# Gate and value projections: two 64-row matmuls on the two row halves of TensorE in place of two 128-row matmuls

## The chip, the cores and the metric

The kernel runs on one core of one Trainium2 chip. The metric is the device time of one execution in microseconds. Three runs of the kernel before took 503.9, 504.02 and 505.62 us; their median is 504.02 us.

## The reference, cut to what matters

```python
x  = attention(q, k, v, i_gate, f_gate, o_gate)   # 1536 tokens x 320, a gated linear attention, chunk by chunk
xn = x / rms(x) * rms_g
g  = xn @ w_gate                                  # 320 x 1536
val = xn @ w_val                                  # 320 x 1536
x  = (g * sigmoid(g) * val) @ w_out               # 1536 x 320
h  = x @ w_in                                     # 320 x 2048
y  = (max(h, 0) + alpha * min(h, 0)) @ w_out2     # 2048 x 320
```

The contraction of the projections is 320 long: two blocks of 128 rows and a remainder of 64 rows. The kernel keeps float32 precision with operands rounded to fp32r: each operand is split into a rounded ("high") part and what is left ("low"), and high x high, high x low and low x high are summed in PSUM. Low x low may be left out.

## The kernel before, in words

The 1536 tokens are worked in four tiles of 384 (`TW`). A tile has an attention part (`ATT`: three groups of 128 tokens, each with the items qT, kT, D0, D1, S, state, inter, intra, norm, scale, xT) and a feed-forward part (`MLP`). `merged()` lays the feed-forward items of tile t and the attention items of tile t+1 into one list; all five engines walk the same list, so the order on TensorE is written out by hand. The first attention tile runs alone (the opening), then three merged tiles, then the last feed-forward part alone.

The feed-forward part of a tile runs over the 12 blocks of 128 hidden columns as gate j, val j, out1 j-1, and then over 16 blocks as in j, out2 j-2. There are thus 4 x 12 = 48 pairs of a gate and its val.

`project` (L964 to 977) makes one such block: eight matmuls of 128 rows x 128 columns against 384 columns of tokens, summed in one PSUM bank (`GV[0]` for gate, `GV[1]` for val). The weights' tile has five blocks. Blocks 0 and 1 are the high parts of the two full 128-row blocks, 2 and 3 their low parts, and block 4 holds the 64-row remainder twice: high part in rows 0 to 63, low part in rows 64 to 127. The tokens' tile `xT[:, part, block, :]` has part 0 high and part 1 low, and its block 2 holds the remainder in both row halves. One pass of block 4 against the high tokens gives high x high and low x high at once. One pass of block 4 against the low tokens gives high x low, which is wanted, and low x low, which is not needed: half of that pass does nothing of use. It is the last of the eight.

After gate j, ScalarE takes the tanh (L532) and VectorE makes `u` (L727); after val j, VectorE makes `hid` (L733), ScalarE rounds it (L510) and GpSimd makes its low part (L845), and `accumulate` (L984, L987) multiplies it by the output weights, nine matmuls of 320 columns. TensorE waits for `s_u` ahead of gate j and for `s_hid` ahead of val j (which frees `GV[1]`).

Between a gate and its val there can be an attention item. In each of the three merged tiles the list puts `gates` behind gate 5 (L891: 8-row matmuls, L894: 40-row transposes), and S behind gate 7 and gate 11 (L928). Item S multiplies `kT` and `qT` for two heads that lie in the two row halves (rows 0 to 39 and rows 64 to 103, the variable `r`), taking turns, eight plain float32 matmuls in all, each of which shows in the trace as two:

```python
for c in range(PAIRS):
    for half in range(2):
        r = HP * half
        last = te.matmul(A[1 - half][:, c * CH:(c + 1) * CH], kT[r:r + D, c, :], qT[r:r + D, c, :], ...)
```

The qT and kT items (L904) are float32 transposes on all 128 rows, 128 columns each.

Of the kernel before, what the change touches and what calls it, by code (L numbers as in the profile page):

```python
# [21 lines left out]
F32 = mybir.dt.float32  # L22
F32R = mybir.dt.float32r
ALU = mybir.AluOpType
# [5 lines left out]
P = 128  # L30
CH = 128
G = 3
TW = G * CH
# [11 lines left out]
NB = DM // P  # L45
REM = DM - NB * P
# [80 lines left out]
def program(nc, q, k, v, i_gate, f_gate, o_gate, w_gate, w_val, w_out, rms_g, w_in, w_out2, alpha, out):  # L127
    ctx = ExitStack()
    with ctx:
        def sb(name, shape, dt=F32):  # L130
            return ctx.enter_context(nc.sbuf_tensor(name, shape, dt))

        def sem(name):
            return ctx.enter_context(nc.semaphore(name))


        wg = sb("wg", [P, 5, FF1], F32R)
        wv = sb("wv", [P, 5, FF1], F32R)
# [13 lines left out]
        xT = sb("xT", [P, 2, XB, TW], F32R)  # L152
# [54 lines left out]
        GV = bank[3:5]  # L207
# [4 lines left out]
        def opening(t):  # L212

            return isinstance(t, int) and t == 0
# [28 lines left out]
        s_wgv_lo = sem("s_wgv_lo")  # L243
# [42 lines left out]
        s_gate_mm = sem("s_gate_mm")  # L286
        s_th1 = sem("s_th1")
        s_u = sem("s_u")
        s_val_mm = sem("s_val_mm")
# [298 lines left out]
        def _(dve):  # L588
            vec = nc.vector
# [176 lines left out]
            def weights(n):  # L766

                if n == EARLY - 1:
                    dve.wait_ge(s_alpha_mm, 1)
                    vec.tensor_copy(alpha_sb[:, :], GV[0][:, 0:J2]).then_inc(s_alpha, 1)  # L770
                if n == 0:
                    return
                n -= 1
                what, c = PIECES[n]
                if what == "o":
                    return
                dve.wait_ge(s_w_hi, n + 1)
                w = wg if what == "g" else wv
                cols = slice(c * SW, (c + 1) * SW)
                src = stage[:, n % NS, :].rearrange("p (a n) -> p a n", a=XB)  # L780
                if what == "g":
                    vec.tensor_tensor(wg[:, NB:2 * NB, cols], src[:, 0:NB], wg[:, 0:NB, cols].bitcast(F32), ALU.subtract)
                vec.tensor_tensor(w[REM:P, 2 * NB, cols], src[REM:P, NB], w[REM:P, 2 * NB, cols].bitcast(F32), ALU.subtract).then_inc(s_wgv_lo, 1)

            tiles(dve, mlp, att, weights)


# [79 lines left out]
        def _(pe):  # L867
            te = nc.tensor
# [9 lines left out]
            def keep(count):  # L878

                for _ in range(count):  # L880
                    te.matmul(quad(GV[1]), identR[:, :], mid(maskR[:, :], P, 4, CH), start=True, stop=True)  # L881
# [79 lines left out]
                        last = te.transpose(xbank(g, t)[:, c * CH:(c + 1) * CH], xn[:, g, c * P:(c + 1) * P], ident[:, :])  # L961
                    last.then_inc(s_x_mm, 1)

            def project(dst, w, x, col, lo=NB, first_of=None, t=None):  # L964


                terms = [(a, 0, a) for a in range(NB)] + [(a, 1, a) for a in range(NB)] + [(lo + a, 0, a) for a in range(NB)]
                terms += [(lo + NB, 0, NB), (lo + NB, 1, NB)]
                terms.sort(key=lambda term: term[1])
                for n, (blk, part, xb) in enumerate(terms):  # L970
                    if part and not terms[n - 1][1]:
                        if first_of == "gate":
                            pe.wait_ge(s_x_lo, BACK + G * t + G)
                        elif first_of == "in":
                            pe.wait_ge(s_x2_lo, G * t + G)
                    last = te.matmul(dst, w[:, blk, col:col + P], x[:, part, xb, :], start=(n == 0), stop=(n == len(terms) - 1))  # L976
                return last

            def accumulate(t, i, w_hi, w_lo, first, final):

                pe.wait_ge(s_hid_hi, BACK + JA * t + i + 1)
                for g in range(G):
                    for m, w in enumerate((w_hi, w_lo)):
                        te.matmul(ACC[g][:, 0:DM], hidT[:, i % NH, 0, g * CH:(g + 1) * CH], w, start=(first and m == 0), stop=False)  # L984
                pe.wait_ge(s_hid_lo, BACK + JA * t + i + 1)
                for g in range(G):
                    last = te.matmul(ACC[g][:, 0:DM], hidT[:, i % NH, 1, g * CH:(g + 1) * CH], w_hi, start=False, stop=final)  # L987
                    if final and g < G - 1:
                        last.then_inc(s_acc_mm, 1)
                last.then_inc(s_out_mm, 1)  # L990

            def mlp(what, j, t):
                if what == "gate":
                    if j * P % SW == 0:
                        pe.wait_ge(s_w_hi, AT[("v", j * P // SW)] + 1)
                        pe.wait_ge(s_wgv_lo, 2 * (j * P // SW) + 2)
                        pe.wait_ge(s_wv_lo, j * P // SW + 1)
                    if j == 0:
                        if opening(t):
                            keep(KEEP_GATE)  # L1000
                        pe.wait_ge(s_alpha, 1)
                        pe.wait_ge(s_x_hi, G * t + G)
                        pe.wait_ge(s_hid, BACK + JA * t)
                    else:
                        pe.wait_ge(s_u, BACK + J1 * t + j)
                    project(GV[0][:, 0:TW], wg, xT, j * P, NB, "gate" if j == 0 else None, t).then_inc(s_gate_mm, 1)
                elif what == "val":
                    if j:
                        pe.wait_ge(s_hid, BACK + JA * t + j)
                    project(GV[1][:, 0:TW], wv, xT, j * P).then_inc(s_val_mm, 1)  # L1010
                elif what == "out1":
                    if j % SJ == 0:
                        pe.wait_ge(s_w_hi, AT[("o", j // SJ)] + 1)
                        pe.wait_ge(s_wo_lo, j // SJ + 1)
                    if j == 0:
                        pe.wait_ge(s_y_act, BACK + 2 * t)
                        pe.wait_ge(s_y_dve, BACK + t)
                    accumulate(t, j, wo[:, 0, j, :], wo[:, 1, j, :], j == 0, j == J1 - 1)
                elif what == "x2T":
                    for g in range(G):  # L1020
                        pe.wait_ge(s_x2_dve, 2 * t + 2) if g == 1 else pe.wait_ge(s_x2_act, 4 * t + g + 2)
                        for c in range(XB):
                            last = te.transpose(X2BANK[g][:, c * CH:(c + 1) * CH], tok[:, g, c * P:(c + 1) * P], ident[:, :])
                        last.then_inc(s_x2T_mm, 1)
                elif what == "in":
                    pe.wait_ge(s_win_lo, J2 * t + j + 1)
                    if j == 0:
                        pe.wait_ge(s_x2_hi, G * t + G)
                        pe.wait_ge(s_x2_lo, G * t + 1)
                    elif j >= 2:  # L1030
                        pe.wait_ge(s_hid, BACK + JA * t + J1 + j - 1)
                    project(GV[j % 2][:, 0:TW], win[:, j % 2], x2T, 0, XB, "in" if j == 0 else None, t).then_inc(s_in_mm, 1)
                elif what == "out2":
                    pe.wait_ge(s_w2_lo, BACK + J2 * t + j + 1)
                    accumulate(t, J1 + j, w2[:, j % 2, 0], w2[:, j % 2, 1], j == 0, j == J2 - 1)

            def weights(n):
                if n == EARLY - 1:
                    pe.wait_ge(s_consts_in, 16 * (2))
                    te.transpose(GV[0][:, 0:J2], alpha_rows[:, :], ident[0:J2, 0:J2]).then_inc(s_alpha_mm, 1)  # L1040

            tiles(pe, mlp, att, weights)


# [20 lines left out]
```

## Time and profile before

| | |
|---|---|
| median of three runs | 504.02 us |
| the profiled execution | 505.44 us |
| its span | 503.6 us |
| outside the span | 1.84 us |
| TensorE matmul busy | 482.7 us (96%), 3161 matmuls |
| VectorE / GpSimd / ScalarE busy | 317.4 / 233.9 / 212.7 us |
| gate and val matmuls (L976, `wg` and `wv`) | 384 + 384 |

In the profile PE is the TensorE matmul and PEld its weight load, which lies beside the matmuls. A matmul's shown duration holds its way through the array, so that durations of neighbours overlap; what a pass occupies is read from one start to the next. In the page's slices each digit is the busy share of a fortieth of the span, in tenths.

### The profile page before, as it was taken

To read this page: it belongs to the slowest core of one execution; us is meant where nothing else is said; L and a number is where in the kernel's file an instruction comes from. 1 tells how busy PE (TensorE), PEld (TensorE's weight loads), DVE (VectorE), ACT (ScalarE), POOL (GpSimd) and SP (SyncE) were. 2 spreads that over 40 slices of the span, in tenths; PEclk is the share of its full clock that TensorE was granted. 3 is DMA by queue.
4 is the path that set the end of the run, shared out by engine and by line. 5 is a ranking of instruction groups with operands and counts; after the bars stand their busy time and mean duration, and the time that the engine had idled before them with its cause. 6 is when DMAs were issued, how large, how long until landed. Compare 5 with 4: busy or idle time off the path is not lost.

```text
span 503.6 us, 9124 instructions
## 1 busy us (share of the span) xinstructions
PE 482.7 (96%) x3161; PEld 463.4 (92%) x3161; DVE 317.4 (63%) x643; ACT 212.7 (42%) x508; POOL 233.9 (46%) x250
## 2 busy tenths in 40 slices
PE   5998989999999999999999999999999999998996
PEld 3887978998999999998999999999899999988996
DVE  7585897657787474449678556438779622236663
ACT  1441536245635324236545423234654422245552
POOL 3540748535657326143746334340855522225673
PEclk9998999999999999999999999999999999999999
DMA  6768332123434680003344390002342320004562
GB/s 112 163 135 176 105 103 75 44 59 98 119 85 116 113 119 2 2 0 74 121 96 91 115 167 1 1 2 56 93 117 81 90 66 0 1 5 114 135 126 97
DMA packets 80729, 41.23 MB, mean 82 GB/s; under 512 B 51548, under 2 KB 80684, under 8 KB 80684
## 3 DMA queue, kind: packets, MB, share of 16 engines
q1 hardware_dynamic: 80684, 40.65, 36.2%
q8 instruction: 26, 0.43, 0.4%
q14 instruction: 19, 0.16, 0.1%
HBM read 38.67 MB, written 1.97 MB: 81 GB/s over the span
## 4 chain that ended last, share of the span: by engine, by line
PE 78%; DVE 12%; issue 3%; POOL 3%; ACT 3%; ACTq 0%; POOLq 0%; DVEq 0%
PE bank L976 38%; PE bank L984 16%; PE bank L987 8%; PE bank L940 4%; PE bank L928 3%; PE bank L904 2%; PE bank L881 2%; PE bank L935 2%; POOL w L837 1%; DVE u L750 1%; PE bank L946 1%; DVE xn L711 1%; PE bank L918 1%; PE bank L919 1%; DVE win L720 1%
## 5 line engine op out<-in xcount | busy, mean ns | idle before, releaser
L845 POOL TENSOR_TENSOR hidT<-hid,hidT 128x384 fp32r<-128x384 f32 x112 | 118.3, 1057 | 227.7 <-ACT hidT L510 227.4
L510 ACT CAST hidT<-hid 128x384 fp32r<-128x384 f32 x112 | 57.5, 513 | 131.5 <-DVE hid L733 93.8
L976 PE MATMUL bank<-x2T,win 128*128 128x384 f32 x512 | 100.2, 339 | 1.2 <-ACT x2T L551 0.8
L976 PEld LDWEIGHTS bank<-x2T,win 128*128 128x128 f32 x512 | 87.6, 188 | 2.9 <-DVE win L720 1.3
L727 DVE SCALAR_TENSOR_TENSOR u<-th,bank 128x384 f32<-128x384 f32 x48 | 26.6, 554 | 92.0 <-ACT th L532 91.9
L976 PE MATMUL bank<-xT,wg 128*128 128x384 f32 x384 | 76.4, 342 | 1.8 <-DVE u L727 1.8
L976 PE MATMUL bank<-xT,wv 128*128 128x384 f32 x384 | 76.3, 341 | 0.0
L984 PE MATMUL bank<-w,hidT 128*128 128x320 f32 x384 | 68.2, 313 | 4.1 <-POOL w L837 3.5
L976 PEld LDWEIGHTS bank<-xT,wg 128*128 128x128 f32 x384 | 67.1, 191 | 2.9 <-issue 2.0
L976 PEld LDWEIGHTS bank<-xT,wv 128*128 128x128 f32 x384 | 66.7, 189 | 1.2 <-DVE hid L733 0.4
L984 PEld LDWEIGHTS bank<-w,hidT 128*128 128x128 f32 x384 | 59.2, 188 | 6.9 <-POOL w L837 5.7
L750 DVE TENSOR_SCALAR u<-bank,alpha_sb 128x384 f32<-128x384 f32 x64 | 39.4, 616 | 38.7 <-PE bank L976 38.1
L837 POOL TENSOR_TENSOR w<-shared,w 128x320 fp32r<-128x320 f32 x60 | 55.9, 932 | 4.5 <-ACT w L526 4.4
L984 PE MATMUL bank<-wo,hidT 128*128 128x320 f32 x288 | 50.9, 312 | 0.0
L532 ACT ACTIVATE th<-bank 128x384 f32<-128x384 f32 x48 | 23.6, 491 | 57.2 <-PE bank L976 57.2
L720 DVE TENSOR_TENSOR win<-shared,win 128x384 fp32r<-128x384 f32 x64 | 41.9, 659 | 7.8 <-ACT win L518 7.8
L984 PEld LDWEIGHTS bank<-wo,hidT 128*128 128x128 f32 x288 | 44.6, 188 | 0.7 <-ACT hidT L510 0.2
L517 ACT CAST win<-shared 128x256 fp32r<-128x256 f32 x64 | 25.9, 405 | 41.7 <-PE bank L976 36.0
L987 PE MATMUL bank<-w,hidT 128*128 128x320 f32 x192 | 38.5, 309 | 0.0
L753 DVE SCALAR_TENSOR_TENSOR hid<-bank,u 128x384 f32<-128x384 f32 x64 | 35.7, 558 | 2.2
L733 DVE SCALAR_TENSOR_TENSOR hid<-u,bank 128x384 f32<-128x384 f32 x48 | 26.5, 552 | 14.2 <-PE bank L976 11.8
L526 ACT CAST w<-shared 128x320 fp32r<-128x320 f32 x64 | 29.1, 455 | 4.7 <-PE bank L987 3.2
(126 smaller groups left out, 631.4 us busy)
## 6 DMA issues: line engine op xcount, KB each, us to landing
shared<-in_moe_w_out SPq DMA_DIRECT2D x38, 320.0 KB, 4.9
shared<-in_moe_w_in SPq DMA_DIRECT2D x34, 256.0 KB
shared<-in_moe_w_in SPq DMA_DIRECT2D x34, 128.0 KB
q_in<-in_q SPq DMA_DIRECT2D x12, 160.0 KB, 4.4
k_in<-in_k SPq DMA_DIRECT2D x12, 160.0 KB, 4.8
v_in<-in_v SPq DMA_DIRECT2D x12, 160.0 KB, 4.8
o_in<-in_o_gate SPq DMA_DIRECT2D x12, 160.0 KB, 4.4
shared<-in_moe_w_gate SPq DMA_DIRECT2D x6, 256.0 KB
```

What stands on the lines that cost most here:

```text
L510: a.copy(hidT[:, i % NH, 0], hid[:, i % 2]).then_inc(s_hid_hi, 1)
L526: a.copy(w2[:, p, 0], w2_raw[:, pair, p]).then_inc(s_w2_hi, 1)
L720: vec.tensor_tensor(win[:, p, XB:2 * XB], win_raw[:, pair, :, cols], win[:, p, 0:XB].bitcast(F32), ALU.subtract).then_inc(s_win_lo, 1)
L727: vec.scalar_tensor_tensor(u[:, :], th1[:, :], 1.0, GV[0][:, 0:TW], ALU.add, ALU.mult).then_inc(s_u, 1)
L733: vec.scalar_tensor_tensor(hid[:, p], u[:, :], 0.5, GV[1][:, 0:TW], ALU.mult, ALU.mult).then_inc(s_hid, 1)
L750: vec.tensor_scalar(u[:, :], GV[p][:, 0:TW], 0.0, alpha_sb[:, j:j + 1], ALU.min, ALU.mult).then_inc(s_leak, 1)
L753: vec.scalar_tensor_tensor(hid[:, p], GV[p][:, 0:TW], 0.0, u[:, :], ALU.max, ALU.add).then_inc(s_hid, 1)
L837: gp.tensor_tensor(w2[:, p, 1], w2_raw[:, pair, p], w2[:, p, 0].bitcast(F32), ALU.subtract).then_inc(s_w2_lo, 1)
L845: gp.tensor_tensor(hidT[:, i % NH, 1], hid[:, i % 2], hidT[:, i % NH, 0].bitcast(F32), ALU.subtract).then_inc(s_hid_lo, 1)
L976: last = te.matmul(dst, w[:, blk, col:col + P], x[:, part, xb, :], start=(n == 0), stop=(n == len(terms) - 1))
L984: te.matmul(ACC[g][:, 0:DM], hidT[:, i % NH, 0, g * CH:(g + 1) * CH], w, start=(first and m == 0), stop=False)
L987: last = te.matmul(ACC[g][:, 0:DM], hidT[:, i % NH, 1, g * CH:(g + 1) * CH], w_hi, start=False, stop=final)
```

## The change

The remainder of `w_val` is stored with its halves swapped: high part in rows 64 to 127, low part in rows 0 to 63 (only the slice of the subtraction that makes the low part changes). The pass of low tokens against block 4 is then replaced in both projections by a matmul of 64 rows that holds the high part alone: rows 0 to 63 for gate, rows 64 to 127 for val. The two are issued one behind the other, gate's as the last of the gate group (`halves="close"`), val's as the first of the val group, and the wait for `s_hid` stands ahead of val's. The rest of val has seven matmuls (`halves="open"`). Low x low of the remainder is no longer summed.

```diff
-                vec.tensor_tensor(w[REM:P, 2 * NB, cols], src[REM:P, NB], w[REM:P, 2 * NB, cols].bitcast(F32), ALU.subtract).then_inc(s_wgv_lo, 1)
+                low = slice(REM, P) if what == "g" else slice(0, REM)
+                vec.tensor_tensor(w[low, 2 * NB, cols], src[low, NB], w[low, 2 * NB, cols].bitcast(F32), ALU.subtract).then_inc(s_wgv_lo, 1)
...
-            def project(dst, w, x, col, lo=NB, first_of=None, t=None):
+            def project(dst, w, x, col, lo=NB, first_of=None, t=None, halves=None):
...
                 terms.sort(key=lambda term: term[1])
+                if halves is not None:
+                    terms.pop()
...
-                    last = te.matmul(dst, w[:, blk, col:col + P], x[:, part, xb, :], start=(n == 0), stop=(n == len(terms) - 1))
+                    last = te.matmul(dst, w[:, blk, col:col + P], x[:, part, xb, :], start=(n == 0 and halves != "open"), stop=(n == len(terms) - 1 and halves != "close"))
+                if halves == "close":
+                    last = te.matmul(dst, w[0:REM, lo + NB, col:col + P], x[0:REM, 1, NB, :], start=False, stop=True)
                 return last
...
-                    project(GV[0][:, 0:TW], wg, xT, j * P, NB, "gate" if j == 0 else None, t).then_inc(s_gate_mm, 1)
-                elif what == "val":
+                    project(GV[0][:, 0:TW], wg, xT, j * P, NB, "gate" if j == 0 else None, t, "close").then_inc(s_gate_mm, 1)
                     if j:
                         pe.wait_ge(s_hid, BACK + JA * t + j)
-                    project(GV[1][:, 0:TW], wv, xT, j * P).then_inc(s_val_mm, 1)
+                    te.matmul(GV[1][:, 0:TW], wv[REM:P, 2 * NB, j * P:(j + 1) * P], xT[REM:P, 1, NB, :], start=True, stop=False)
+                elif what == "val":
+                    project(GV[1][:, 0:TW], wv, xT, j * P, halves="open").then_inc(s_val_mm, 1)
```

The two lists below are TensorE's instructions in the first merged tile, in program order. In the changed kernel the lines are numbered anew: L979 is the 128-row matmul of `project` (L976 before), L981 gate's half pass, L1014 val's half pass, L989 and L992 are `accumulate` (L984, L987 before), L929 is S (L928 before). The first place is a gate with its val and nothing between them. Before:

```order
L976 MATMUL bank<-xT,wg 128x384 [waits s_u]
L976 MATMUL bank<-xT,wg 128x384 x7
L976 MATMUL bank<-xT,wv 128x384 [waits s_hid]
L976 MATMUL bank<-xT,wv 128x384 x7
L984 MATMUL bank<-wo,hidT 128x320 [waits s_hid_hi,s_wo_lo,s_w_hi]
L984 MATMUL bank<-wo,hidT 128x320 x5
```

The same place in the changed kernel:

```order
L979 MATMUL bank<-xT,wg 128x384 [waits s_u]
L979 MATMUL bank<-xT,wg 128x384 x6
L981 MATMUL bank<-xT,wg 128x384
L1014 MATMUL bank<-xT,wv 128x384 [waits s_hid]
L979 MATMUL bank<-xT,wv 128x384 x7
L989 MATMUL bank<-wo,hidT 128x320 [waits s_hid_hi,s_wo_lo,s_w_hi]
```

Sixteen matmuls of 128 rows have become fourteen with two of 64 rows in their middle, and the wait for `s_hid` has moved with val's first matmul. The second place is gate 7 with S behind it, before:

```order
L976 MATMUL bank<-xT,wg 128x384 [waits s_u]
L976 MATMUL bank<-xT,wg 128x384 x7
L928 MATMUL bank<-qT,kT 128x128 [waits s_dx,s_kT,s_qT]
L928 MATMUL bank<-qT,kT 128x128 x7
L976 MATMUL bank<-xT,wv 128x384 [waits s_hid]
L976 MATMUL bank<-xT,wv 128x384 x7
```

And in the changed kernel:

```order
L979 MATMUL bank<-xT,wg 128x384 [waits s_u]
L979 MATMUL bank<-xT,wg 128x384 x6
L981 MATMUL bank<-xT,wg 128x384
L1014 MATMUL bank<-xT,wv 128x384 [waits s_hid]
L929 MATMUL bank<-qT,kT 128x128 [waits s_dx,s_kT,s_qT]
L929 MATMUL bank<-qT,kT 128x128 x7
L979 MATMUL bank<-xT,wv 128x384 x7
```

Here the two 64-row matmuls stand directly ahead of S, and val has lost one matmul behind it. ScalarE's and SyncE's instructions are the same as before; on VectorE and GpSimd the order is unchanged.

## Rows read from the trace of the kernel before

**Rows 1.** The page: busy time of TensorE, and its slices over the span.

```profile
PE 482.7 (96%) x3161; PEld 463.4 (92%) x3161; DVE 317.4 (63%) x643; ACT 212.7 (42%) x508; POOL 233.9 (46%) x250
...
PE   5998989999999999999999999999999999998996
...
PEclk9998999999999999999999999999999999999999
```

**Rows 2.** The page: the chain that ended last, by engine.

```profile
PE 78%; DVE 12%; issue 3%; POOL 3%; ACT 3%; ACTq 0%; POOLq 0%; DVEq 0%
```

**Rows 3.** Who TensorE's matmuls waited for: total us, times, longest us.

```profile
PE bank L876 <- DVE maskR L607: 5.4, 1, 5.4
PE bank L984 <- POOL w L837: 3.5, 7, 0.7
...
PE bank L976 <- DVE u L727: 1.8, 1, 1.8
...
PE bank L928 <- ACT dx L497: 0.5, 1, 0.5
```

**Rows 4.** Timeline of PE, a gate and val alone: start us, us, line, shapes, count.

```profile
300.03 1.55 PE L976 MATMUL bank<-xT,wg 128*128 128x384 f32 x8
301.42 1.55 PE L976 MATMUL bank<-xT,wv 128*128 128x384 f32 x8
302.81 1.03 PE L984 MATMUL bank<-wo,hidT 128*128 128x320 f32 x6
```

**Rows 5.** Timeline of PE, gate 9 and val 9 with transposes between and behind.

```profile
211.02 1.55 PE L976 MATMUL bank<-xT,wg 128*128 128x384 f32 x8
212.41 0.60 PE L904 MATMUL bank<-ident,q_in 128*104 128x128 f32 x4
212.76 1.63 PE L976 MATMUL bank<-xT,wv 128*128 128x384 f32 x8
214.22 0.60 PE L904 MATMUL bank<-ident,k_in 128*104 128x128 f32 x4
```

**Rows 6.** Timeline of PE, gate 7 and val 7 with S between.

```profile
198.10 1.55 PE L976 MATMUL bank<-xT,wg 128*128 128x384 f32 x8
199.58 1.16 PE L928 MATMUL bank<-qT,kT 40*128 40x128 f32 x16
200.67 1.67 PE L976 MATMUL bank<-xT,wv 128*128 128x384 f32 x8
202.18 0.30 PE L984 MATMUL bank<-wo,hidT 128*128 128x320 f32 x1
```

**Rows 7.** Timeline of PEld inside S of another tile: the last 14 of 16 loads.

```profile
105.73 0.86 PEld L928 LDWEIGHTS bank<-qT,kT 40*128 40x128 f32 x14
```

**Rows 8.** Groups by line: busy us, mean ns, idle before and its releaser.

```profile
L976 PEld LDWEIGHTS bank<-xT,wv 128*128 128x128 f32 x384 | 66.7, 189 | 1.2 <-DVE hid L733 0.4
...
L727 DVE SCALAR_TENSOR_TENSOR u<-th,bank 128x384 f32<-128x384 f32 x48 | 26.6, 554 | 92.0 <-ACT th L532 91.9
...
L532 ACT ACTIVATE th<-bank 128x384 f32<-128x384 f32 x48 | 23.6, 491 | 57.2 <-PE bank L976 57.2
...
L928 PEld LDWEIGHTS bank<-qT,kT 40*128 40x128 f32 x192 | 11.7, 187 | 3.7 <-issue 3.7
```

**Rows 9.** Timeline of PE, gate 5 and val 5 with `gates` between.

```profile
187.24 1.55 PE L976 MATMUL bank<-xT,wg 128*128 128x384 f32 x8
188.72 0.42 PE L891 MATMUL bank<-vals_rhs,mstack 8*128 8x48 f32 x2
189.07 0.38 PE L894 MATMUL bank<-ident,gt 40*128 40x40 f32 x3
189.37 1.66 PE L976 MATMUL bank<-xT,wv 128*128 128x384 f32 x8
190.87 0.60 PE L904 MATMUL bank<-ident,q_in 128*104 128x128 f32 x4
```

## The prediction

> **What bounds the kernel now.** I read the page first. TensorE is busy 96% of the span, its slices show nines nearly throughout, and its granted clock is nine tenths of the full 2.4 GHz or more in all slices but one [rows 1]. A busy share can mislead, since shown durations overlap, so the chain of waits comes second: 78% of the path that ended last is TensorE's own work [rows 2]. Third, the list of what TensorE waited for: 5.4 us once at the very start, 3.5 us in seven pieces in the out2 stage, and in the gate and val stage one single wait of 1.8 us, for `u` [rows 3]. So in the stage that the change touches TensorE runs from one instruction to the next. Each nanosecond taken from or added to its stream there goes to the end, apart from what that one wait can swallow.
>
> **What a pass costs.** The timeline gives it by starts. Gate starts at 300.03, its val at 301.42, the out1 matmuls at 302.81 [rows 4]: sixteen passes in 2.78 us, 0.1738 us each. The eight loads of each half are hidden: nothing stands between the matmuls.
>
> **What the change removes.** In each of 48 pairs two full passes go, 2 x 0.1738 = 0.347 us. In their place come two 64-row passes on different row halves.
>
> **Do two such passes overlap?** Item S does the same thing with 40 rows in each half. Inside S fourteen loads, seven pairs, take from the first start to the last end 0.86 us, and one load lasts 0.187 us [rows 7, 8]. So six pair intervals take 0.86 - 0.187 = 0.67 us, 0.112 us a pair. A float32 pass of 128 columns on all rows costs 0.087 us by one bracket and 0.109 by another: the four transposes start at 212.41 and val at 212.76, and the same bracket taken whole, 214.22 - 211.02 - 2.78 = 0.42 us, gives 0.105 us each [rows 5]. I take the whole bracket, since the start of a first matmul behind a change is shown early. Two passes of S in 0.112 us against 0.105 for one: the halves run side by side. For 384 columns I take one full pass plus the excess of 0.112 over 0.105, 0.174 + 0.007 = 0.181 us. The bounds are one pass (0.174) and two (0.347).
>
> **What does the step to half rows and back cost?** The trace of before has no 64-row fp32r matmul, but S stands between a gate and its val, so its bracket can be compared with the others. With nothing between: 2.78 us. With transposes on all rows between: 3.20, and the 0.42 is their own work [rows 5], so a switch to another type of operand and back costs nothing that shows. With S between: 202.18 - 198.10 = 4.08 us [rows 6]. Less 2.78 for gate and val, less 8 x 0.112 = 0.90 for S's eight pairs, 0.40 us are left that are nobody's work. They can be seen at both ends. Gate's eight passes should end at 198.10 + 1.39 = 199.49, and S shows its first start at 199.58. Before each S the loads stood idle, 3.7 us in twelve S, 0.31 us each, put down to "issue", not to any engine [rows 8]: in the plain stream a load is always pulled ahead, here it is not. Behind S, val's eight matmuls need 202.18 - 200.67 = 1.51 us in place of 1.39. That matches an array that is emptied when it goes from 128-row use to half rows, and again on the way back, with the first weight load exposed each time. Semaphores are not the reason: the wait list has S waiting once, for 0.5 us [rows 3], and the transposes also follow a wait.
>
> The Trainium skill's page "TensorEngine Tiling (Array Packing)", section "Key Properties", has the rule that changing the tiling mode drains TensorE while changing the tile within a mode does not; it gives no price. By that rule, the trace agrees: 0.40 us a round trip around S and nothing between the pairs inside it.
>
> **The sum.** A pair that stands alone among 128-row passes: -0.347 + 0.181 + 0.40 = +0.234 us. Two round trips' worth of ends are paid for one saved pass; I take S's price unchanged, since the gate passes ahead of it and the val passes behind it are the very ones that the new pair will stand between.
>
> - 39 pairs have 128-row matmuls on both sides: 39 x 0.234 = +9.1 us.
> - 6 pairs (gate 7 and gate 11 in three merged tiles) stand directly ahead of S. There the step is paid today already and is shared: -0.347 + 0.181 = -0.166 each, -1.0 us. Bounds: -0.166 if shared, +0.234 if 64 rows and 40 rows count as different.
> - 3 pairs (gate 5) stand ahead of `gates`, which has 8-row and 40-row matmuls. Its bracket, 190.87 - 187.24 - 2.78 = 0.85 us for five tiny passes [rows 9], shows that it pays for steps too, and 8 rows are not the same cut of the array as 64. Shared or not is open, between -0.166 and +0.234; I take the upper, +0.7 us, as nearest, since the two 8-row passes and the 40-row ones behind them already cost more than S's pairs each.
> - The wait of 1.8 us for `u` in the first merged tile is VectorE being late, not TensorE [rows 3]. A longer stretch ahead of it shortens it: about one pair, -0.2 us.
> - The wait for `s_hid` now stands ahead of the half pass, one pass earlier than before, and where an attention item lies between gate and val, ahead of that item. All loads of val together waited 0.4 us for `hid` [rows 8], and `hid` of block j-1 is made while TensorE has out1 and gate still to do (nine passes of 320 columns and eight of 384), so nothing: 0 us. If that cover were gone, the half pass and S behind it would stand for `hid`.
> - gate's end comes some 0.2 us later to ScalarE and VectorE. `u` is needed by val's end, 1.4 us on; `th` and `u` take 0.49 and 0.55 [rows 8]. Hidden, 0 us.
> - VectorE's changed slice has the same size: 0 us. No DMA and no wait of a queue is touched.
>
> Together +9.1 - 1.0 + 0.7 - 0.2 = **+8.6 us**. The profiled execution has a span of 503.6 and 1.84 outside it; with the sum it would be 512.2 and 514.0. It lies 1.4 above the median of 504.02, so against the median I expect 504.02 + 8.6 = **512.6 us**, 1.7% slower.
>
> The main case has bounds of its own. Low: `gates` shared (-1.2), a round trip of 0.37 in place of 0.40 (-1.3), 0.8 more swallowed by the wait: 509.3. High: S not shared (+2.4), 0.44 a round trip (+1.6), wait swallows nothing (+0.2): 516.8.
>
> **Rivals.**
>
> *Free steps (faster).* What S pays belongs to S alone, to plain float32 on few rows, or hides behind a longer pass: 384 columns keep the array busy 0.174 us where S's pass has 0.105, so a load pulled ahead could be covered. Then each pair costs 0.181: 48 x -0.166 = -8.0, 496.0 us. For it: the pairs inside S run at full overlap. Against it: the shown start of S comes late behind a 384-column pass already, so the long pass covers nothing; and the float32 transposes pay nothing. It decides where the round trip falls under 0.166 us. The page "TensorE: Matmul & The Clock Gate" of the Trainium skill, in "Measured speedup vs the span model", counts a packed set as one matmul plus about 4 ns per tile and no step; by it alone the change gains. Chance 0.09.
>
> *Half the step.* Part of the 0.40 is S's own (the second pair's load behind an empty array, which 384 columns may cover), and only some 0.2 remains: 39 x (-0.347 + 0.181 + 0.2) = +1.3, with the six shared pairs +0.3, 504.3 us. Nothing in the rows splits off such a part; chance 0.06.
>
> *Steps and no overlap.* The two half passes run one behind the other, because fp32r takes its columns faster (384 in 0.174 us, where S's float32 has 128 in 0.105) or because the semaphore between them breaks the pair. Then 48 x 0.167 = +8.0 on top: 520.6 us. Against it: nothing in S's rows shows such a limit. Chance 0.07.
>
> *The change does not take hold*, the half passes use the whole array: two full passes as before and no steps, 504 us. Against it: S's operands lie in the same two halves and do overlap. Chance 0.02.
>
> The main case has 0.76.
>
> **How the numbers follow.** A measurement of this kernel can tell about 0.5% (2.5 us) from no change. Faster by more: 0.09. Within: half the step and no hold, 0.08. Slower: 0.76 + 0.07 = 0.83. The range must leave out no more than 0.2. The main case's own range is 509.3 to 516.8; out of it fall the free steps, half the step, no hold (0.17 together) and the tails, so I reach up over the no-overlap case and down a little: 508.0 to 521.5.
>
> **What would show it.** In the changed profile: L981 and L1014 start some 7 ns apart (the excess of a pair above); L981 shows its start some 0.26 us behind the pass before it, and the load ahead of it an idle time put down to issue, some 0.3 us x 42 = 13 us in all; a gate and val alone take 3.01 us from gate's start to out1's start in place of 2.78; gate, S and val take 3.91 in place of 4.08. The idle time of val's loads for `hid` stays under 1 us. The prediction is wrong if a gate and val alone take under 2.78 us (free steps), about 2.8 (half), or 3.2 (no overlap).

## The result and the profile after

The changed kernel took 512.02 us (median of four runs, 510.43 to 512.02), the kernel before beside it 504.45 us (503.9 to 505.62). The ratio is 1.0145 with a 95% interval of 1.0128 to 1.0162: slower by 1.5%. The forecast was 512.6 us in a range of 508.0 to 521.5, and slower with a chance of 0.83. One run of the kernel before, beside e5 below, took 951.68 us where its sixteen neighbours took 503.87 to 505.69, and it is left out of every comparison.

The profiled execution has a span of 510.2 us, 6.6 more than before. The page's lines that answer to [rows 1] and [rows 2]:

```profile
PE 491.4 (96%) x3161; PEld 454.3 (89%) x3161; DVE 316.8 (62%) x643; ACT 213.1 (42%) x508; POOL 233.6 (46%) x250
...
PE   5998989999999999999999999999999999998996
...
PEclk9998999999999999999999999999999999999999
...
PE 82%; DVE 10%; POOL 3%; issue 3%; ACT 2%; ACTq 0%; POOLq 0%; DVEq 0%
```

The count of matmuls is the same, and so are the slices of TensorE, whose busy time is 8.7 us longer. The weight loads' busy time is 9.1 us shorter, though their count is the same: the two 64-row loads of a pair lie over each other, 0.18 us in each of 48 pairs, and count once. The busy times of VectorE, ScalarE and GpSimd moved by less than 1 us. This is a change in TensorE's stream alone.

The timeline of TensorE for a gate and val with nothing between them, the answer to [rows 4], first its matmuls, then its weight loads (start us, us, line, shapes, count; in brackets the idle time before and its releaser):

```profile
298.89 1.38 PE L979 MATMUL bank<-xT,wg 128*128 128x384 f32 x7
300.19 0.44 PE L981 MATMUL bank<-xT,wg 64*128 64x384 f32 x1
300.20 0.44 PE L1014 MATMUL bank<-xT,wv 64*128 64x384 f32 x1
300.57 1.48 PE L979 MATMUL bank<-xT,wv 128*128 128x384 f32 x7
301.89 1.03 PE L989 MATMUL bank<-wo,hidT 128*128 128x320 f32 x6
```

```profile
300.19 0.18 PEld L981 LDWEIGHTS bank<-xT,wg 64*128 64x128 f32 x1 [0.25 <-issue]
300.20 0.18 PEld L1014 LDWEIGHTS bank<-xT,wv 64*128 64x128 f32 x1
300.57 1.16 PEld L979 LDWEIGHTS bank<-xT,wv 128*128 128x128 f32 x7 [0.19 <-issue]
```

From gate's start to out1's start it is 301.89 - 298.89 = 3.00 us, where it was 2.78. The two 64-row matmuls start 0.01 us apart, so they do overlap. But the load of the first comes only after an idle 0.25 us, and the first 128-row load behind them after another 0.19. Both pauses are put down to "issue": no engine and no DMA is behind them. Over all 48 pairs the first pause is this group of the list by line:

```profile
L981 PEld LDWEIGHTS bank<-xT,wg 64*128 64x128 f32 x48 | 8.8, 183 | 12.0 <-issue 12.0
```

The same stretch with S between gate and val, the answer to [rows 6]:

```profile
200.12 1.38 PE L979 MATMUL bank<-xT,wg 128*128 128x384 f32 x7
201.43 0.44 PE L981 MATMUL bank<-xT,wg 64*128 64x384 f32 x1
201.44 0.44 PE L1014 MATMUL bank<-xT,wv 64*128 64x384 f32 x1
201.72 1.05 PE L929 MATMUL bank<-qT,kT 40*128 40x128 f32 x16
202.70 1.49 PE L979 MATMUL bank<-xT,wv 128*128 128x384 f32 x7
204.03 1.03 PE L989 MATMUL bank<-wo,hidT 128*128 128x320 f32 x6
```

204.03 - 200.12 = 3.91 us in place of 4.08. Here the change does what it says: a pass is saved, and no pause is added, since the one ahead of S was there before. With `gates` between, the answer to [rows 9]:

```profile
189.01 1.38 PE L979 MATMUL bank<-xT,wg 128*128 128x384 f32 x7
...
190.69 0.42 PE L892 MATMUL bank<-vals_rhs,mstack 8*128 8x48 f32 x2
...
192.67 0.60 PE L905 MATMUL bank<-ident,q_in 128*104 128x128 f32 x4
```

192.67 - 189.01 = 3.66 us in place of 3.63. The three kinds of place differ by one pause each: +0.22, +0.03, -0.17. These numbers are the same in every tile behind the first merged one, to within 0.05 us.

### The profile page after: what moved, and what is told of

The parts are those of the page before. It is cut to its first block, busy times and chain, and to the rows that moved or that the text cites. A ratio compares the mean times of both kernels' runs of the same rounds, so it can differ in the third digit from the quotient of the medians.

```text
span 510.2 us, 9124 instructions
## 1 busy us (share of the span) xinstructions
PE 491.4 (96%) x3161; PEld 454.3 (89%) x3161; DVE 316.8 (62%) x643; ACT 213.1 (42%) x508; POOL 233.6 (46%) x250
## 4 chain that ended last, share of the span: by engine, by line
PE 82%; DVE 10%; POOL 3%; issue 3%; ACT 2%; ACTq 0%; POOLq 0%; DVEq 0%
PE bank L979 36%; PE bank L989 16%; PE bank L992 8%; PE bank L941 4%; PE bank L981 3%; PE bank L929 2%; PE bank L882 2%; PE bank L905 2%; PE bank L936 2%; POOL w L838 1%; DVE u L750 1%; PE bank L947 1%; DVE xn L711 1%; PE bank L919 1%; PE bank L920 1%
## 5 line engine op out<-in xcount | busy, mean ns | idle before, releaser
L979 PE MATMUL bank<-x2T,win 128*128 128x384 f32 x512 | 100.2, 339 | 1.2 <-ACT x2T L551 0.8
L979 PEld LDWEIGHTS bank<-x2T,win 128*128 128x128 f32 x512 | 87.6, 188 | 2.9 <-DVE win L720 1.3
L989 PE MATMUL bank<-w,hidT 128*128 128x320 f32 x384 | 68.2, 313 | 4.1 <-POOL w L838 3.5
L979 PE MATMUL bank<-xT,wv 128*128 128x384 f32 x336 | 71.1, 351 | 0.0
L979 PE MATMUL bank<-xT,wg 128*128 128x384 f32 x336 | 67.1, 339 | 1.2 <-DVE u L727 1.2
L989 PEld LDWEIGHTS bank<-w,hidT 128*128 128x128 f32 x384 | 59.2, 188 | 6.9 <-POOL w L838 5.7
L979 PEld LDWEIGHTS bank<-xT,wv 128*128 128x128 f32 x336 | 55.9, 188 | 7.0 <-issue 6.2
L979 PEld LDWEIGHTS bank<-xT,wg 128*128 128x128 f32 x336 | 58.0, 189 | 2.4 <-issue 1.4
L989 PE MATMUL bank<-wo,hidT 128*128 128x320 f32 x288 | 50.9, 312 | 0.0
L989 PEld LDWEIGHTS bank<-wo,hidT 128*128 128x128 f32 x288 | 44.7, 188 | 0.7 <-ACT hidT L510 0.2
L992 PE MATMUL bank<-w,hidT 128*128 128x320 f32 x192 | 38.5, 309 | 0.0
```

## The experiments

**Theory A**: each change between 128-row use of the array and half rows costs some 0.20 us, and the only saving is one pass of 0.17 us. **Rivals**: B, the new order (val's first pass and its wait tied to gate's end) costs something; C, what costs is the pair of short passes, not the change; D, the halves don't overlap and the change is cheaper; E and F stand with their kernels. The measure is the stretch from gate's start to out1's start in the timeline, which is 2.78 us before and 3.00 in the changed kernel. The expectations give it from gate's start to the next gate's, which is 1.31 us longer (4.09 and 4.31), since the nine matmuls of out1 are in it. Runs e2, e3, e4 and e6 were timed once each, so they are read by their stretches first and by their times second.

**e1, full rows in the new order.**

```diff
-                    last = te.matmul(dst, w[0:REM, lo + NB, col:col + P], x[0:REM, 1, NB, :], start=False, stop=True)
+                    last = te.matmul(dst, w[:, lo + NB, col:col + P], x[:, 1, NB, :], start=False, stop=True)
...
-                    te.matmul(GV[1][:, 0:TW], wv[REM:P, 2 * NB, j * P:(j + 1) * P], xT[REM:P, 1, NB, :], start=True, stop=False)
+                    te.matmul(GV[1][:, 0:TW], wv[:, 2 * NB, j * P:(j + 1) * P], xT[:, 1, NB, :], start=True, stop=False)
```

> Both half passes take all 128 rows again (the remainder's low x low is summed again), in the changed kernel's order, with the wait for s_hid ahead of val's first pass. Theory A (all of the cost is the change between 128-row and half-row use of the array, 0.20 us each way, less the pass that is saved): no extra cost is left, gate to gate with nothing but out1 between takes 4.09 us as in the kernel before, and the time is that of the kernel before within 0.3%. Rival B (a part of the cost is the order: val's first pass and its wait tied to gate's end): gate to gate stays above 4.09, and the time 1 to 8 us above the kernel before.

Measured: ratio to the kernel before 0.9998 (0.9982 to 1.0014), median 504.94 us, range 503.32 to 505.72. The timeline of a plain stretch:

```profile
294.18 1.38 PE L979 MATMUL bank<-xT,wg 128*128 128x384 f32 x7
295.40 0.34 PE L981 MATMUL bank<-xT,wg 128*128 128x384 f32 x1
295.57 0.34 PE L1014 MATMUL bank<-xT,wv 128*128 128x384 f32 x1
...
296.96 1.03 PE L989 MATMUL bank<-wo,hidT 128*128 128x320 f32 x6
```

2.78 us. Order, moved wait and swapped storage cost nothing; rival B falls. All that is left is the two passes' rows.

**e2, one half pass.** As e1, but gate's pass keeps its 64 rows.

```diff
-                    te.matmul(GV[1][:, 0:TW], wv[REM:P, 2 * NB, j * P:(j + 1) * P], xT[REM:P, 1, NB, :], start=True, stop=False)
+                    te.matmul(GV[1][:, 0:TW], wv[:, 2 * NB, j * P:(j + 1) * P], xT[:, 1, NB, :], start=True, stop=False)
```

> Only gate's pass is cut to 64 rows; val's first pass takes all 128 rows. Nothing overlaps, one pass is as long as another, and each plain pair has one step down and one back. Theory A: gate to gate 4.09 + 0.40 = 4.49 us; pairs ahead of S unchanged (the step is shared); in all 39 x 0.40 + 3 x 0.20 = +16.2 us less at most 1.8 swallowed, some 519 to 521 us. Rival C (what costs is the pair, two short passes whose loads do not hide, and a single one costs half of it): 4.3 us or less, and under +9 us in all.

Measured: 521.73 us. The weight loads of a plain stretch:

```profile
305.39 0.18 PEld L981 LDWEIGHTS bank<-xT,wg 64*128 64x128 f32 x1 [0.25 <-issue]
305.76 0.19 PEld L1014 LDWEIGHTS bank<-xT,wv 128*128 128x128 f32 x1 [0.19 <-issue]
```

and its matmuls:

```profile
304.09 1.38 PE L979 MATMUL bank<-xT,wg 128*128 128x384 f32 x7
...
307.26 1.03 PE L989 MATMUL bank<-wo,hidT 128*128 128x320 f32 x6
```

307.26 - 304.09 = 3.17 us, 0.39 over the plain stretch: the round trip by itself, with the same number of passes as before. A single half pass costs all of it, so rival C falls. One part of the expectation was wrong: it called the pairs ahead of S unchanged and gave those ahead of `gates` one change. In this kernel val's full pass stands between gate's half pass and the item, so nothing is shared. The stretch with S rose from 4.08 to 4.46 us (203.16 to 207.62), the one with `gates` from 3.63 to 4.02. Together that is 2.9 us more than expected. This run also has in it the fall of the clock described in the last section, which is worth some 1.5 us. The time of 521.7 lies over the expected 519 to 521 by less than these two, since some 2 us were swallowed by waits.

**e3, both half passes on rows 0 to 63.** The remainder of `w_val` is stored as in the kernel before.

```diff
-                low = slice(REM, P) if what == "g" else slice(0, REM)
+                low = slice(REM, P)
...
-                    te.matmul(GV[1][:, 0:TW], wv[REM:P, 2 * NB, j * P:(j + 1) * P], xT[REM:P, 1, NB, :], start=True, stop=False)
+                    te.matmul(GV[1][:, 0:TW], wv[0:REM, 2 * NB, j * P:(j + 1) * P], xT[0:REM, 1, NB, :], start=True, stop=False)
```

> Both half passes on rows 0 to 63, one behind the other; the remainder of w_val is stored as in the kernel before. One round trip as in the changed kernel, but no two row halves at once. Theory A (the halves overlap fully, a round trip costs 0.40): the second pass shows, gate to gate 4.31 + 0.17 = 4.49 us, pairs ahead of S as in the kernel before, some +16 us in all. Rival D (no overlap in the changed kernel and a cheaper round trip of 0.23 us): 4.31 us as in the changed kernel, and its time, 512 us.

Measured: 519.88 us. The timeline of a plain stretch:

```profile
302.98 1.38 PE L979 MATMUL bank<-xT,wg 128*128 128x384 f32 x7
304.29 0.44 PE L981 MATMUL bank<-xT,wg 64*128 64x384 f32 x1
304.57 0.33 PE L1014 MATMUL bank<-xT,wv 64*128 64x384 f32 x1
...
306.17 1.03 PE L989 MATMUL bank<-wo,hidT 128*128 128x320 f32 x6
```

306.17 - 302.98 = 3.19 us, 0.19 more than in the changed kernel, and the second half pass now starts 0.28 us behind the first and not 0.01. In the changed kernel the two do run side by side, at nearly the price of one; rival D falls.

**e4, two round trips in each pair.** One of val's full passes is put between the halves (and left out of the seven behind).

```diff
+                if halves == "open":
+                    terms.pop(0)
...
-                    te.matmul(GV[1][:, 0:TW], wv[REM:P, 2 * NB, j * P:(j + 1) * P], xT[REM:P, 1, NB, :], start=True, stop=False)
+                    te.matmul(GV[1][:, 0:TW], wv[:, 0, j * P:(j + 1) * P], xT[:, 0, 0, :], start=True, stop=False)
+                    te.matmul(GV[1][:, 0:TW], wv[REM:P, 2 * NB, j * P:(j + 1) * P], xT[REM:P, 1, NB, :], start=False, stop=False)
```

> One of val's 128-row passes is put between the two half passes, so that each plain pair has two round trips and no overlap. Theory A: the price is linear in changes, gate to gate 4.09 + 4 x 0.20 = 4.89 us; pairs ahead of S have two changes more, +0.40, those ahead of the gates item three, +0.60; in all 31.2 + 2.4 + 1.8 = +35 us less at most 2 swallowed, 537 to 540 us. Rival C (the cost hangs on the pair, or is paid once for both steps when they come close): 4.5 us or less, under 522 us.

Measured: 536.05 us. The weight loads of a plain stretch (L983 gate's half pass, L1016 val's full pass, L1017 val's half pass, L981 the rest of val):

```profile
312.21 0.18 PEld L983 LDWEIGHTS bank<-xT,wg 64*128 64x128 f32 x1 [0.25 <-issue]
312.58 0.19 PEld L1016 LDWEIGHTS bank<-xT,wv 128*128 128x128 f32 x1 [0.19 <-issue]
312.95 0.18 PEld L1017 LDWEIGHTS bank<-xT,wv 64*128 64x128 f32 x1 [0.18 <-issue]
313.32 1.00 PEld L981 LDWEIGHTS bank<-xT,wv 128*128 128x128 f32 x6 [0.19 <-issue]
```

and the two ends of the stretch:

```profile
310.90 1.38 PE L981 MATMUL bank<-xT,wg 128*128 128x384 f32 x7
...
314.48 1.03 PE L991 MATMUL bank<-wo,hidT 128*128 128x320 f32 x6
```

314.48 - 310.90 = 3.58 us, 0.80 over the plain stretch: four pauses, four changes, 0.20 us each. The price is linear, even when the changes stand one pass apart. The stretches of all pairs, the first merged tile's waits set apart, add up to +34.9 us, as expected. The whole fell 1 us short of 537: against e1's trace, which like this one has no fall of the clock, the span is 32.4 us longer, so the waits swallowed some 2.5 us and not the 2 allowed for.

**e6, gate's last pass with 96 rows.** As e1, with one slice changed (rows 64 to 95 add half of the remainder's low x low).

```diff
-                    last = te.matmul(dst, w[:, lo + NB, col:col + P], x[:, 1, NB, :], start=False, stop=True)
+                    last = te.matmul(dst, w[0:96, lo + NB, col:col + P], x[0:96, 1, NB, :], start=False, stop=True)
```

> As the kernel with full rows in the new order, but gate's last pass takes rows 0 to 95 (the remainder's high x low and half of its low x low). Theory A (what costs is cutting the array into row halves, not a pass with fewer than 128 rows): nothing is paid, as with the 104-row passes of the kernel before; gate to gate 4.09 us and some 504 us in all. Rival F (any pass with other rows than its neighbours pays): 4.49 us and some 520 us, as with one half pass.

Measured: 503.66 us, and no pause:

```profile
294.18 1.38 PE L979 MATMUL bank<-xT,wg 128*128 128x384 f32 x7
295.39 0.34 PE L981 MATMUL bank<-xT,wg 96*128 96x384 f32 x1
...
296.96 1.03 PE L989 MATMUL bank<-wo,hidT 128*128 128x320 f32 x6
```

2.78 us. This kernel differs from e2's in one slice alone, 96 rows in place of 64: a pass with fewer rows than its neighbours is free at 96 and costs 0.39 at 64. Rival F falls: the price hangs on the cut into row halves. Where between 64 and 96 it begins wasn't tried.

**e5, half passes only ahead of S.** The changed kernel, with 64 rows only where S is the next item (gate 7 and gate 11 of the merged tiles).

```diff
+S_BEHIND = [a[1][1] for a, b in zip(MERGED, MERGED[1:]) if a[1][0] == "gate" and b[1][0] == "S"]
...
-                    last = te.matmul(dst, w[0:REM, lo + NB, col:col + P], x[0:REM, 1, NB, :], start=False, stop=True)
+                    last = te.matmul(dst, w[0:rows_, lo + NB, col:col + P], x[0:rows_, 1, NB, :], start=False, stop=True)
...
-                    project(GV[0][:, 0:TW], wg, xT, j * P, NB, "gate" if j == 0 else None, t, "close").then_inc(s_gate_mm, 1)
+                    at_S = j in S_BEHIND and t != NT - 1
+                    project(GV[0][:, 0:TW], wg, xT, j * P, NB, "gate" if j == 0 else None, t, "close", REM if at_S else P).then_inc(s_gate_mm, 1)
...
-                    te.matmul(GV[1][:, 0:TW], wv[REM:P, 2 * NB, j * P:(j + 1) * P], xT[REM:P, 1, NB, :], start=True, stop=False)
+                    own = slice(REM if at_S else 0, P)
+                    te.matmul(GV[1][:, 0:TW], wv[own, 2 * NB, j * P:(j + 1) * P], xT[own, 1, NB, :], start=True, stop=False)
```

> Half passes only at gate 7 and gate 11 of the three merged tiles, directly ahead of S; all other pairs take 128 rows as before. Theory A (each change of use costs 0.20 us, and ahead of S no change is added): the six stretches are each 0.17 to 0.18 us shorter, as in the changed kernel, the other 42 as in the kernel before; in all 1.1 us less, 0.2% faster, which lies at the edge of what can be told from no change. Rival E (in the changed kernel those six gained only because the array was used by halves all the time): the six stretches do not shrink, and the time is that of the kernel before or above it.

Measured: ratio to the kernel before 0.9974 (0.996 to 0.9988), median 503.54 us, the kernel before beside it 505.16 (sixteen runs). Its stretch with S:

```profile
195.92 1.38 PE L980 MATMUL bank<-xT,wg 128*128 128x384 f32 x7
...
197.52 1.05 PE L930 MATMUL bank<-qT,kT 40*128 40x128 f32 x16
...
199.83 1.03 PE L990 MATMUL bank<-wo,hidT 128*128 128x320 f32 x6
```

3.91 us as in the changed kernel, where the kernel before has 4.08. This version beats the kernel before by 0.26%: the interval leaves out 1, though the gain is smaller than the 1.6 us by which runs of one kernel differ. The traces bear it out in the main. Against e1, whose other stretches are the same, five of the six stretches with S are 0.17 us shorter. In the sixth, gate 7 of the first merged tile, S waits for `dx`, and the stretch is as long as in e1 (4.49 and 4.48 us). That makes 0.87 us of the 1.1 between the two spans; the rest is mostly a shorter wait for `u` (1.41 us against 1.65) ahead of the first of these places, which the half passes can't have caused. A saved pass with no change of use added is a gain, and rival E falls.

The changes counted, with c = 0.20 us for one change and the 0.17 us saved where two halves overlap. For each place: the changes added, and what its stretch measured over that of the kernel before (gate 5, `gates` and val 5: 3.63 us before, 4.02 in e2, 3.83 in e3, 4.23 in e4; gate, S and val in e4: 4.47):

```
place                    changed kernel        e2             e3             e4
gate, val                2c - 0.17 = +0.22     2c = +0.39     2c = +0.41     4c = +0.80
gate, S, val              0 - 0.17 = -0.17     2c = +0.38     0 =  0.00      2c = +0.39
gate, gates, val          c - 0.17 = +0.03     2c = +0.39     c = +0.20      3c = +0.60
```

One price fits all twelve to within 0.02 us.

## Why the prediction was right

**The bound.** That TensorE's stream is the path, so that each pause in it goes to the end, held: the stretches' differences add up to the difference of the spans, below.

**The pass and the overlap.** 0.1738 us a pass and 0.181 for an overlapped pair were right: the two half passes start 3 to 4 ns apart in 46 of 48 pairs (7 forecast), the stretch with S fell by 0.17, as forecast (3.91 us forecast and measured), and e3 shows the second pass when the overlap is taken away.

**The price of the step.** Read off S's bracket as 0.40 us a round trip; e2 measured 0.39 and e4 0.80 for two. The plain stretch was forecast at 3.01 us and came out at 3.00. (The prediction's words "two round trips' worth of ends" say too much: its sum has one round trip, with its two ends, and that is what e2 shows.) The idle time ahead of L981's loads was forecast at 13 us and is 12.0, but that is near by luck: it was taken as 0.3 us in 42 pairs and is 0.25 us in all 48, since the pause ahead of S now stands ahead of the half pass. Taking a 40-row float32 item as the price list for 64-row fp32r passes was sound. The Trainium skill's "TensorEngine Tiling (Array Packing)", "Key Properties", says that a change of the mode drains TensorE and a change of tile within it does not. The traces agree with both halves: 0.20 us a change (e4), and 0.01 us between the two half passes. The rival by the Trainium skill's "TensorE: Matmul & The Clock Gate", "Measured speedup vs the span model", counts a packed set as one matmul and about 4 ns per tile. The traces agree with it inside the mode only, with 3 to 4 ns from one half pass to the other; it has no term for the 0.39 us of the way in and out.

**The 39 plain pairs.** Forecast +9.1 us. Most stretches from gate to gate grew by 0.23, those of gate 1, gate 8 and gate 9 mostly by 0.18 to 0.21; by the starts of the gates in both traces they come to +8.55, the first merged tile's waits and the clock set apart.

**The 6 pairs ahead of S.** Forecast -1.0, measured -1.04: sharing was the right choice.

**The 3 pairs ahead of `gates`.** Forecast +0.7 by the upper bound, measured +0.08. The step that failed is the choice of the upper end. From 64 to 8 rows is one more change, as I argued, but the way back from the item to 128 rows was paid before and stays one: a single c, not a round trip, c - 0.17 = +0.03, and e3 shows the c by itself at this place (+0.20). Half-way between the bounds would have been right.

**The wait in the first merged tile.** Forecast -0.2, measured -1.16. The list of waits of the kernel before has for this tile (46 to 112 us)

```profile
PE bank L904 <- DVE gt_tok L654: 0.6, 1, 0.6
```

and the list of the changed kernel, the answer to [rows 3],

```profile
PE bank L979 <- DVE u L727: 1.2, 1, 1.2
...
PE bank L905 <- DVE gt_tok L654: 0.2, 1, 0.2
```

The wait for `u` shrank from 1.8 to 1.2, and two waits that I had not counted shrank as well. The one for `gt_tok` went from 0.62 to 0.25. (The changed kernel's list also lacks a wait of 0.5 us for `gt_tok` in the opening, but there the matmul behind it starts at 12.71 us against 12.70, so nothing came of it.) The one for `dx` is gone from the list, but only 0.20 us of it was swallowed: S's stretch behind gate 7 fell from 4.67 to 4.30 us, where the others fell by 0.17. VectorE's late work moves less than TensorE does: the last out1 matmuls ahead of the wait for `u` start 1.09 us later than before (63.20 us against 62.11), the gate behind it only 0.48 us later (64.97 against 64.49). So each such wait swallows pauses gathered ahead of it. How much is not sharp, since the same wait differs by 0.24 us between e1 and e5, whose TensorE programs are the same up to there. This term was mis-sized by 1.0 us.

**The sum.** The first gate of the first merged tile comes where the clock falls (last section). The second gate starts at 50.67 us against 50.29 before, 0.38 later, of which its pair explains 0.22; the other 0.16 I put to the clock. Then 8.55 - 1.04 + 0.08 - 1.16 + 0.16 = 6.6 us, and the spans differ by 6.6; the forecast sum was 8.6. So it was 2 us too high: 0.6 in the plain pairs, 0.6 ahead of `gates`, 1.0 in the waits, less the 0.16 of the clock. It is no merit of the sum that the forecast time lies only 0.6 us from the median. The changed kernel has runs at two times, 510.43 and 512.02. So has the kernel before in the main, 503.9 and 505.5 (thirteen runs beside e1: seven from 503.89 to 503.97, six from 505.45 to 505.75), though of the other twenty runs five lie between, from 504.31 to 504.9. I measured from 504.02, a lower value, and the median after is an upper one. Like for like the change costs 6.5 us, 1.3%. That is at the lower end of the interval of the ratio, and inside the range either way.

## What to carry to other kernels

Cutting the array into row halves pays by the visit, not by the pass: a visit costs 0.39 us here and a pair of 384-column passes in it saves 0.17, so by these two numbers it takes three such pairs in one visit to gain anything (that was not tried). Look for places where the visit is paid already, as ahead of S, and put the half-row work there. The price of a change can be read before making it: take two brackets of the same stretch, one with the foreign item between and one without, and subtract the item's own steady pitch.

## What the runs showed that I had not expected

One thing that moves the time by over 1 us without any change to the kernel lies behind the opening. The view by stretches (us, busy times of PE, PEld, DVE, ACT and POOL, then the granted clock of TensorE and DMA) has for the kernel before

```profile
46.00:47.50 1.50, 1.50 (x6) 1.41 (x6) 0.07 (x1) 0.00 (x0) 0.00 (x0) 0.50 0.91 295
47.50:49.00 1.50, 1.50 (x7) 1.50 (x6) 0.00 (x0) 0.09 (x1) 0.00 (x0) 0.50 0.32 61
```

and for e1, whose profiled execution took 503.65 us,

```profile
46.00:47.50 1.50, 1.50 (x11) 1.46 (x10) 0.20 (x1) 0.00 (x0) 0.00 (x0) 1.00 1.00 309
47.50:49.00 1.50, 1.50 (x10) 1.40 (x9) 0.56 (x1) 0.49 (x1) 0.00 (x0) 1.00 0.37 71
```

In the one the first gate runs at the lower level of 1.2 GHz, in the other at 2.4, with 13 matmuls against 21 in the same 3 us. From the first gate to the second the one trace has 4.18 us and the other 2.78, that is 1.4 of the 1.7 us between their spans. Ahead of it TensorE had stood idle for 2.0 us in both, waiting for `xn`. The changed kernel's profiled execution, at 512.02, has the fall too, a little earlier: 0.65 of full speed in 44 to 46 us, 0.50 in 46 to 47.5, 0.83 in 47.5 to 49. So have e2's and e3's; those of e4, e5 and e6 have not. This fits the two times, but it doesn't settle them: the mean granted clock of a run does not sort the runs of the kernel before (0.995 at 503.93 us, 0.996 at 505.75). What decides whether the fall comes wasn't looked into.

In e3, with both half passes on rows 0 to 63 and S behind them, the order of starts is not the program's:

```profile
204.13 0.44 PE L981 MATMUL bank<-xT,wg 64*128 64x384 f32 x1
204.14 0.48 PE L929 MATMUL bank<-qT,kT 40*128 40x128 f32 x2
204.41 0.34 PE L1014 MATMUL bank<-xT,wv 64*128 64x384 f32 x1
204.59 1.05 PE L929 MATMUL bank<-qT,kT 40*128 40x128 f32 x14
```

L1014 comes ahead of S (L929) in the program, but its row half is the one that L981 holds. Two records of S start ahead of it, by 0.27 and 0.06 us. The rows don't say which half of S they are; if they are those on rows 64 to 103, as I take them to be, a matmul on a free row half does not wait for an earlier one on the busy half. Nothing is gained by it here: e3's stretch with S takes 4.08 us (202.82 to 206.90), 0.17 more than in the changed kernel, so the second half pass costs its full price at this place too.
